# Retention and two mixture-of-experts layers on one core: the split w1 operands in rows of another pitch

## The reference

```python
for e in range(E):
    h = np.maximum(x @ w1[e], 0.0)      # 1536 x 512 times 512 x 1024
    out += P[:, e:e + 1] * (h @ w2[e])  # 1536 x 1024 times 1024 x 512
```

## Time and profile before

| what | before |
|---|---|
| median of 3 runs | 1552.88 us |
| the profiled execution: its time | 1552.96 us |
| the profiled execution: first to last instruction (span) | 1551.2 us |
| TensorE matmul busy | 1543.7 us |
| VectorE busy | 880.9 us |
| ScalarE busy | 445.2 us |
| GpSimd busy | 53.8 us |

### The profile page before, as it was taken

One profiled execution on the slowest core, in us unless ns is written; L12 is line 12 of the kernel. 1 busy time (PEld: TensorE's weight loads), 2 busy tenths in 40 slices (PEclk: granted clock), 3 DMA queues, 4 the chain that ended last, 5 costly groups with the idle time before them and its releaser, 6 DMA issues.

```text
span 1551.2 us, 21289 instructions
## 1 busy us (share of the span) xinstructions
PE 1543.7 (100%) x8238; PEld 1401.2 (90%) x8238; DVE 880.9 (57%) x1439; ACT 445.2 (29%) x860; POOL 53.8 (3%) x45
## 2 busy tenths in 40 slices
PE   8999999999999999999999999999999999999999
PEld 7989988998899889988998899889998999899988
DVE  6756855546546555465465555567555556555553
ACT  5422331322223213222232132243332223213321
POOL 5300000000000000000000000012000000000000
PEclk9999999999999999999999999999999999999999
DMA  9201101001011010010110100101101001011011
GB/s 341 78 1 55 55 2 55 28 28 55 1 54 54 0 54 27 27 54 2 52 54 0 54 29 26 55 0 55 51 4 55 28 28 55 0 54 54 1 41 68
DMA packets 34891, 67.28 MB, mean 43 GB/s; under 512 B 2320, under 2 KB 2704, under 8 KB 34832
## 3 DMA queue, kind: packets, MB, share of 16 engines
q1 hardware_dynamic: 34400, 66.42, 12.5%
q10 hardware_dynamic: 432, 0.04, 0.0%
HBM read 63.31 MB, written 3.15 MB: 43 GB/s over the span
## 4 chain that ended last, share of the span: by engine, by line
PE 98%; DVE 1%; DMA 0%; SPq 0%; ACT 0%; issue 0%; DVEq 0%
PE bank L1148 17%; PE bank L1149 17%; PE bank L1147 17%; PE bank L1126 15%; PE bank L1130 15%; PE bank L1128 15%; PE bank L999 1%; PE bank L1019 1%; PE bank L1037 1%; PE bank L1031 0%; DVE w_lo L667 0%; DMA qt_in<-in_q_t 0%; PE bank L1090 0%; DVE w_hi L722 0%; DVE x_sum L636 0%; PE bank L1071 0%
## 5 line engine op out<-in xcount | busy, mean ns | idle before, releaser
L1126 PE MATMUL bank<-x_hi,w_hi 128*128 128x384 f32 x1344 | 449.9, 335 | 0.4 <-DVE ups L805 0.4
L1130 PE MATMUL bank<-x_hi,w_lo 128*128 128x384 f32 x1344 | 449.5, 334 | 0.0
L1128 PE MATMUL bank<-x_lo,w_hi 128*128 128x384 f32 x1344 | 449.2, 334 | 0.0
L1149 PE MATMUL bank<-w_hi,h_lo 128*128 128x512 f32 x1148 | 447.6, 390 | 0.0
L1148 PE MATMUL bank<-w_lo,h_hi 128*128 128x512 f32 x1148 | 447.4, 390 | 0.0
L1147 PE MATMUL bank<-w_hi,h_hi 128*128 128x512 f32 x1148 | 446.9, 389 | 0.0
L852 DVE SCALAR_TENSOR_TENSOR acc<-bank,gate,acc 128x512 f32<-128x512 f32 x251 | 188.5, 751 | 372.7 <-PE bank L1149 372.7
L538 ACT COPY ups<-bank 128x384 f32<-128x384 f32 x288 | 138.0, 479 | 902.8 <-PE bank L1130 902.7
L805 DVE TENSOR_TENSOR ups<-bank,ups 128x384 f32<-128x384 f32 x288 | 155.4, 555 | 190.1 <-ACT ups L538 168.4
L1149 PEld LDWEIGHTS bank<-w_hi,h_lo 128*128 128x128 f32 x1148 | 215.4, 188 | 44.9
L1148 PEld LDWEIGHTS bank<-w_lo,h_hi 128*128 128x128 f32 x1148 | 215.4, 188 | 43.8
(11 more groups left out here) (96 smaller groups left out, 508.4 us busy)
## 6 DMA issues: line engine op xcount, KB each, us to landing
w_raw<-in_moe_w SPq DMA_DIRECT2D x46, 1024.0 KB, 5.0
kt_in<-in_k_t SPq DMA_DIRECT2D x12, 256.0 KB, 3.9
qt_in<-in_q_t SPq DMA_DIRECT2D x12, 256.0 KB, 5.2
v_in<-in_v SPq DMA_DIRECT2D x12, 256.0 KB, 5.6
k_in<-in_k SPq DMA_DIRECT2D x10, 256.0 KB, 5.4
out<-acc SPq DMA_DIRECT2D x2, 768.0 KB, 3.5
out<-acc SPq DMA_DIRECT2D x5, 256.0 KB, 2.0
w_raw<-in_moe_w SPq DMA_DIRECT2D x4, 256.0 KB, 5.6
```

The lines of the kernel that those rows point to most:

```text
L1126: nc.tensor.matmul(o, w1_hi[:, w, kc, fs], x_hi[:, x, kc, at], start=start and kc == 0, stop=False, skip_group_check=True)
L1128: nc.tensor.matmul(o, w1_hi[:, w, kc, fs], x_lo[:, x, kc, at], start=False, stop=False, skip_group_check=True)
L1130: last = nc.tensor.matmul(o, w1_lo[:, w, kc, fs], x_hi[:, x, kc, at], start=False, stop=kc == 1, skip_group_check=True)
L1149: last = nc.tensor.matmul(o, h_lo[:, f, b, rows], w2_hi[:, f, :], start=False, stop=(n == UC - 1))
```

## The change

`w1_hi` and `w1_lo` get padded rows. The part of one operand for one half of K stays 256 values long, but the next one begins 260 values later (`W1_ROW`), and 16 more values stand behind the two. Behind each of the two tensors stands a filler of 24 values. The code that uses `w1_hi` and `w1_lo` is the same: it now gets a view of the padded rows.

```diff
+W1_ROW = 2 * P + 4
...
-        w1_hi = sb("w1_hi", [P, 7, 2, 2 * P], F32R)
-        w1_lo = sb("w1_lo", [P, 7, 2, 2 * P], F32R)
+
+        w1_hi_rows = sb("w1_hi", [P, 7, 2 * W1_ROW + 16], F32R)
+        sb("w1_place0", [P, 24])
+        w1_lo_rows = sb("w1_lo", [P, 7, 2 * W1_ROW + 16], F32R)
+        sb("w1_place1", [P, 24])
+
+        def w1_parts(rows):
+            return rows[:, :, 0:2 * W1_ROW].rearrange("p m (k f) -> p m k f", k=2)[:, :, :, 0:2 * P]
+
+        w1_hi, w1_lo = w1_parts(w1_hi_rows), w1_parts(w1_lo_rows)
         w1_sum = sb("w1_sum", [P, 3, 2, 2 * P])
```

## The result

The changed kernel takes 1558.7 us (median of four runs, 1558.58 to 1559.13) against 1552.88 us of the kernel before, measured beside it (four runs, 1552.81 to 1552.95). The ratio is 1.0037 with the 95% interval 1.0025 to 1.0049: **slower by 0.37%**, 5.8 us. That lies inside the predicted range of 1539 to 1567 and outside the likeliest case. The profiled execution took 1558.58 us, with a span of 1556.8, 5.6 us more than before.

A forecast was written before the change was run, and what follows sets the result against it. The prediction took TensorE's distance from matmul to matmul as the bound. All terms were zero: the profiled 1552.96 us plus 0, set 0.08 lower to the median of the runs, gave 1552.9 us, range 1539 to 1567.

The forecast's parts named there:

- the likeliest case: Whole kernel: rate unchanged, by itself 1552.4 to 1553.5 us; chance 0.56, slower splits in the first unit included.
- What bounds the kernel: TensorE: only the distance between two matmuls, or a new wait of TensorE, can move the time.
- Down keeps its rate: Down of the loop: x, w2 and h keep their remainders, so a down takes 16.36 us again.
- Price of a load at another remainder: The 4032 weight loads of up: taken as zero, with bounds of 53.8 us gain and 13.7 us cost.
- rival B: Matmul steps of up: new remainders clash with the moving stream, slower, 1566.6 us at 3.4 ns a load; chance 0.20.
- The unsettled heads: First steps of an up or down: overhead about 3 to 4 ns higher behind a switch, then it settles; cause unknown.
- Rival A: Loads of up: the common remainder costs now, its removal gains, 1539.2 us at modest size, 1499.1 at full; chance 0.24.
- The splits: Operand writes on DVE and ACT: broken runs cost nothing, splits stay at 1216 to 1218 and 1037 to 1045 ns.
- the first unit: Splits of w1 in the chain before TensorE's wait at 63.7 us: zero, bound 0.5 us either way.
- the queues: Loads, stores and queues: no DMA, wait, semaphore or instruction is added; zero.

## Why the prediction was right or wrong

**What bounds the kernel: right.** TensorE's pitch sets the time, no wait appeared in the loop, and the result is the change of that pitch.

**Down keeps its rate: right for the pitch, and off by 0.02 us a down for the head,** which follows how the up in front ended: down's own operands stand as before, and in the run with w1 at 64 the down behind the up of 176.7 ns takes 16.36 us, the others 16.34. The text had named two signs of being wrong, up's length moved by more than 0.07 us and down's moved at all. Both came: up by 0.14, and down by 48 x 0.02 = 1.0 us in all, the other way than up.

**Price of a load at another remainder: here the likeliest case failed.** The step was "I take zero", on the ground that an overhead that is the same for three lengths and two kinds of tile reads as a fixed cost of changing weights. All those matmuls had lengths that are multiples of 64 columns and starts at one remainder, so the sameness said nothing about a fixed cost; at 248 and 264 columns it is 28 and 24 cycles. And "down, with other tiles, settles at the same overhead" was used against rival B for the same reason, though down's tiles stood at the same remainder. The unsettled heads, which I listed and left without a cause, were the row that could have warned: there the overhead moved with nothing but a switch in front of it. What lies behind heads and remainders no run shows.

**Rival B happened,** with its place (the step between two matmuls of up) and its sign. Its size was given twice too large (the term that was mis-sized): 0.14 us over 84 matmuls are 1.7 ns each, where the row of the heads gave 3.4, so 4032 x 1.7 = 6.7 us in place of 13.7. Its variant, in which only the second halves of K pay, gave 1559.7, close to the 1558.7 measured, and the second halves moved alone gave 1559.2; but its reason (not a multiple of 32) fell with the moves by 64 and 128. The price of 3.4 ns was by chance nearly that of all loads moved by 16, 3.3 ns. It was also read from times of two decimals: in ns the six steps of the head take 1066 for 1040, 4.3 ns each, and 4032 x 4.3 = 17.3 us would have put the upper end near 1570. That the range holds the result is in part luck, since it was sized by a row of which no run says that it has the same cause; in down the same kind of move costs 6.1 to 6.9 ns.

**Rival A** did not happen in any of the kernels that moved w1 or x: no up took less than its 84 matmuls at 173.3 ns, 14.56 us. The 96-byte move gained 0.02 us an up on the unsettled head only, about 1 us in 1553, which its interval does not tell from none. Its idea, that the common remainder costs something, did come true in one place that the change does not touch: 256 columns over moved tiles of down took about 118 ns for 120.0.

**The two rules of the Trainium skill.** The note on cachelines of 16 bytes in the Trainium skill (SBUF — State Buffer) gave 1552.9 us, since no start crosses a line more than before; measured are 5.8 us more, so the number of lines does not account for it. The Trainium skill (TensorE: Matmul & The Clock Gate, Part 2, step 1) says that weight loads take nothing from the running stream, by which the change would do nothing; here moving only the tiles that are loaded, by 16 bytes, made the pitch 176.7 ns for 173.3. The trace does not agree with that for this 4-byte type.

**The splits, the first unit, the queues: right**, 1217 and 1215 ns on DVE and 1032 and 1041 on ACT, the sums at 63.16 us as before at 63.20, no new wait in the loop.

**What stays open** is the mechanism below: the runs show that pitch depends on both starts, on the number of columns and on what ran just before, and that the same remainder (64) has three rhythms. No run shows why, and no theory here gave all the numbers: 1 falls with w1 at 16, 3 with the steps of 96, 2 with 64, and 4 missed the down with h at 96 and the cut at 248. Of the 14 remainders of the changed kernel only 0, 16, 64, 96 and 128 were tried with every operand on them, so its 0.14 us is not added up from single prices. Nor were h and w2 moved together.

## What to carry to other kernels

Where TensorE runs without waits, the byte at which its two operands begin is part of the rate: up to 6.9 ns a matmul here, 1.5% of the kernel, from padding alone. Of the starts that were tried in the loop none beats those of the kernel before clear of the noise, and a common remainder alone does not bring their pitch (14.75 us with both operands at 16). So if something in front of the operands changes size, fill it up to a multiple of 256 bytes, which leaves every start where it was modulo 256, and compare the pitch from start to start before and after. The first four matmuls of the logits show that 256 bytes themselves cost nothing there: their loads begin 256 bytes off those of the rest (`wg_parts[:, c + kc, 64:192]`, in values of 4 bytes), and the four take 0.69 us, 173 ns each, like the others.

```profile
65.97 0.33 PE L1071 MATMUL bank<-x_hi,wg_parts 128*128 128x384 f32 x1
...
66.66 0.33 PE L1071 MATMUL bank<-x_hi,wg_parts 128*128 128x384 f32 x1
```

A quantity that is constant in a trace where nothing varies has no price that can be read from it. The prediction gave both sides a chance, 0.24 and 0.20, and its range holds the result because of that; what had no ground was to take the absence of a price for the likeliest case.

## What the runs showed that I had not expected

- The overhead over one column a cycle is not fixed: 28 and 32 cycles at 248 and 256 columns, 24 at 264 columns (whose stream begins at 224), 40 cycles with w1 at 16 bytes (176.7 ns for 384 columns).
- A move of 96 bytes is free for w1 and 384 columns (14.57 us an up) and costs 0.50 us in the 72 matmuls of h and 512 columns. A move of h by 16 bytes costs 6.1 ns a matmul at 512 columns and gives back about 1.5 at 256.
- Moving both operands by the same 16 bytes does not restore the pitch: 14.75 us against 14.59.
- The same remainder, 64, ran at 173.3, 174.6 and 176.7 ns a matmul in one execution of one kernel, by what had run just before.
